# GpSimd's second-stage sums in pieces by feature block, joint scores from step 8 on, one weight rounding behind a ScalarE copy

## What is computed

```python
scores = (q @ k.T) / sqrt(64);  ret = scores * decay_mask;  x = ret @ v   # 8 batches, 8 heads, 576 positions, 64 wide
h = max(x @ w1, x @ w2, x @ w3)    # 4608 tokens, 512 -> 768
x = h @ w_out                      # 768 -> 512
a, b = x @ u1, x @ u2              # 512 -> 1024
out = (a * b) @ u3 @ u_out         # 1024 -> 512
```

## Time and profile before

| | before |
|---|---|
| median of 3 runs | 1218.41 us |
| profiled execution | 1220.39 us, span 1218.6 us |
| TensorE matmul busy | 1207.2 us, 99% |
| VectorE busy | 740.1 us, 61% |
| ScalarE busy | 487.3 us, 40% |
| GpSimd busy | 438.0 us, 36% |
| DMA | 169.66 MB, mean 139 GB/s |

### The profile page before, as it was taken

One profiled execution on the slowest core, in us unless ns is written; L12 is line 12 of the kernel. 1 busy time (PEld: TensorE's weight loads), 2 busy tenths in 40 slices (PEclk: granted clock), 3 DMA queues, 4 the chain that ended last, 5 costly groups with the idle time before them and its releaser, 6 DMA issues.

```text
span 1218.6 us, 22445 instructions
## 1 busy us (share of the span) xinstructions
PE 1207.2 (99%) x8978; PEld 1182.5 (97%) x8978; DVE 740.1 (61%) x1059; ACT 487.3 (40%) x781; POOL 438.0 (36%) x234
## 2 busy tenths in 40 slices
PE   9999999999999999999999999999999999999999
PEld 8778899999999999999999999999999999999998
DVE  5556748745454454668887776454545456876652
ACT  3434544424232322326555444242424234554451
POOL 3646745220202010063787850202020217366550
PEclk9999999999999999999999999999999999999999
DMA  9999943021212030234564531313131252444441
GB/s 360 330 354 391 310 144 136 29 85 46 78 46 85 33 98 27 83 126 147 174 227 166 169 139 53 111 52 113 57 108 64 95 190 87 155 160 158 163 155 65
DMA packets 87335, 169.66 MB, mean 139 GB/s; under 512 B 9272, under 2 KB 58680, under 8 KB 87232
## 3 DMA queue, kind: packets, MB, share of 16 engines
q1 hardware_dynamic: 87232, 168.24, 39.2%
HBM read 106.33 MB, written 61.87 MB: 138 GB/s over the span
## 4 chain that ended last, share of the span: by engine, by line
PE 95%; issue 2%; DMA 1%; DVE 1%; ACT 0%; SPq 0%; POOL 0%; DVEq 0%; ACTq 0%; POOLq 0%
PE ps L1354 28%; PE ps L1356 28%; PE ps L1355 28%; PE ps L1262 2%; PE ps L1276 1%; PE ps L1206 1%; PE ps L1249 1%; PE ps L1222 1%; PE ps L1280 1%; PE ps L1278 1%; DMA xd<-xst 1%; DMA vs<-vv 0%; PE ps L1177 0%; DMA raw<-hd 0%; DVE probs L1005 0%
## 5 line engine op out<-in xcount | busy, mean ns | idle before, releaser
L1354 PE MATMUL ps<-chi,whi 128*128 128x384 f32 x2016 | 673.9, 334 | 1.2 <-ACT w L985 0.7
L1356 PE MATMUL ps<-chi,wlo 128*128 128x384 f32 x2016 | 673.4, 334 | 0.0
L1355 PE MATMUL ps<-clo,whi 128*128 128x384 f32 x2016 | 673.4, 334 | 0.0
L724 POOL TENSOR_TENSOR raw<-raw,raw 128x768 f32<-128x768 f32 (+3 forms) x102 | 269.2, 2659 | 572.0 <-DMA raw<-xd 203.9
L1354 PEld LDWEIGHTS ps<-chi,whi 128*128 128x128 f32 x2016 | 378.4, 188 | 2.6 <-ACT w L985 1.0
L1355 PEld LDWEIGHTS ps<-clo,whi 128*128 128x128 f32 x2016 | 378.4, 188 | 0.0
L1356 PEld LDWEIGHTS ps<-chi,wlo 128*128 128x128 f32 x2016 | 378.4, 188 | 0.0
L994 DVE TENSOR_TENSOR clo<-raw,chi 128x768 fp32r<-128x768 f32 (+2 forms) x168 | 253.0, 1534 | 33.7 <-ACT chi L903 33.7
L903 ACT CAST chi<-raw 128x768 fp32r<-128x768 f32 (+2 forms) x168 | 180.3, 1082 | 83.9 <-PE ps L1356 51.0
L985 ACT COPY w<-ps 128x384 f32<-128x384 f32 x126 | 60.7, 482 | 240.9 <-PE ps L1356 239.3
L972 ACT COPY u<-ps 128x384 f32<-128x384 f32 x126 | 60.8, 483 | 161.2 <-PE ps L1356 159.6
(11 more groups left out here) (64 smaller groups left out, 796.6 us busy)
## 6 DMA issues: line engine op xcount, KB each, us to landing
gd<-h SPq DMA_DIRECT2D x96, 192.0 KB, 1.9
raw<-gd SPq DMA_DIRECT2D x24, 768.0 KB, 6.0
qks<-qk SPq DMA_DIRECT2D x30, 576.0 KB, 7.0
hd<-h SPq DMA_DIRECT2D x72, 192.0 KB, 1.9
raw<-hd SPq DMA_DIRECT2D x24, 576.0 KB, 5.6
x2d<-h SPq DMA_DIRECT2D x48, 192.0 KB, 2.7
raw<-x2d SPq DMA_DIRECT2D x24, 384.0 KB, 4.1
outT<-h SPq DMA_DIRECT2D x48, 192.0 KB, 1.9
```

The lines of the kernel that those rows point to most:

```text
L724: return nc.gpsimd.tensor_tensor(out_, a, b, op)
L1354: nc.tensor.matmul(to, w1, x1, start=(start and k == 0), stop=False, skip_group_check=True)
L1355: nc.tensor.matmul(to, w1, x2, start=False, stop=False, skip_group_check=True)
L1356: last = nc.tensor.matmul(to, w2, x1, start=False, stop=(k == KH[st] - 1), skip_group_check=True)
```

## The change

Three edits. The last four lines of each `combine` case become a helper, `pieces`, which for every tile of stage C splits each of the four sums into `KH[C]` = 3 instructions of 128x384; for the first tile of stage O the sums i = 2 and 3 stay in four pieces as they were. The semaphore counts up at the last piece. `SINGLE` goes from 4 to 8, so steps 4 to 7 use single scores, and `late_features` keeps a late feature only from step 7 on. The cast of weight 11's second part moves from "p2" to "w", behind the copy `w`.

```diff
+W_HI[11, 1] = (56, "w")
-SINGLE = 4
+SINGLE = 8
-    return features(m)[-1:] if m < STEPS - 2 else []
+    return features(m)[-1:] if SINGLE - 1 <= m < STEPS - 2 else []
+                def pieces(to, a, b):
+                    parts = KH[tau // TILES] if tau // TILES == C or (tau == O * TILES and i >= 2) else 1
+                    for k in range(parts - 1):
+                        add(x(to, k), x(a, k), x(b, k), ALU.subtract)
+                    k = slice(None) if parts == 1 else parts - 1
+                    add(x(to, k), x(a, k), x(b, k), ALU.subtract).then_inc(combined, 1)
-                    add(x(4), x(3), x(0), ALU.subtract).then_inc(combined, 1)
+                    pieces(4, 3, 0)
-                    add(x(1), x(6), x(4), ALU.subtract).then_inc(combined, 1)
+                    pieces(1, 6, 4)
...
+                    pieces(3, 6, 3)
...
+                    pieces(5, 2, 1)
```

## The result

The changed kernel takes 1234.34 us (median of 4 runs, 1233.11 to 1238.11), the kernel before 1218.61 us (4 runs, 1218.19 to 1220.7). The ratio of the runs on record is 1.0122, 95% interval 1.0105 to 1.014: slower, by 14.9 us if the ratio is taken (0.0122 x 1218.6), by 15.7 us if the medians are. The forecast was 1224.8 us, its range ended at 1228.5. The direction was right, the size was not: +15.7 us where +6.4 stood.

The account below looks back on a forecast made before the run. TensorE, 95% of the chain of waits, was taken to bound the kernel. Terms of -0.7 + 7.4 - 0.9 + 0.6 = +6.4 us on 1218.4 gave 1224.8 us; range with the rivals 1216.8 to 1228.5.

Parts of the forecast that it names:

- the chain: Tile 7: third sum ends 2.1 us later, its cast and copy `s` follow on ScalarE, TensorE stalls 1.5 us with restart.
- The turns: GpSimd and VectorE in stage C: the waiting one is served when an instruction ends; one turn costs GpSimd 1.1 us.
- The loop through `h`: Stage C: the next tile's load waits behind copy `h`; rounds become 23.7 us, +5.7 us from tile 8 to 11.
- waits of weights 12 and 13 at `w`: Expected sign in stage C: new TensorE idle times waiting for ScalarE's copy `w` at units 60 and 64.
- tiles 7 to 11, +7.4: Stage C after its first tile: pieces make sums, `s` and `u` late; +1.2 to +10.2 us, taken as +7.4.
- tile 6: First tile of stage C: pieces hold VectorE's op less and remove a 0.5 us idle time and slow restart; -0.7 us.
- Nothing on TensorE's path by my count: First tile of stage C: GpSimd's 11.51 us become some 14, which only weight 10 waits for.
- the cast of weight 11: Unit 56: `w` no longer stands behind this cast, so a 0.7 us idle time and its restart go; -0.9 us.
- the retention: Front of the kernel, `SINGLE` 8 and late features: dearer single scores against fewer stops and less half clock; +0.6 us.
- Step 6's stop: Retention: TensorE's 1.07 us stop, read as a late instruction block, goes because blocks last some 1.3 us longer; -1.07 us.
- Step 4's: Retention: TensorE's 2.44 us stop keeps its place in the stream and hides that step's +1.08 us of single scores; 0.
- The lower end of the turns: Rival for stage C: VectorE's turns fall as before, only the pieces' fixed part is paid; 1218.6 us, chance 0.24.

Follow-up runs that it names:

- scores only: Only `SINGLE` 8 and the late features changed against the kernel before, cast and sums as before: 1221.26 us, ratio 1.0006.
- tile 6 and one more sum: Changed kernel with stage C's pieces only in tile 6 and tile 7's first sum, scores and cast as changed: 1219.87 us, ratio 0.999 to the kernel before.
- cast only: Only the cast of weight 11's second part moved behind the copy `w`, against the kernel before: 1220.01 us, ratio 1.0.
- the reordered kernel: Changed kernel, all pieces kept, position 3's cast behind copy `s` and position 5's behind `h` and `u` in stage C: 1225.42 us, ratio 1.0042.
- only `h` and `u` moved: Changed kernel, all pieces kept, only position 5's cast put behind copies `h` and `u` in stage C: 1225.93 us, ratio 1.0042.

## Why the prediction was wrong in size

**Right: the chain.** The turns, who is queued behind whom, and which copy is late were as worked out. The third sum was foretold to end at 580.6 us and `s` to be there at 582.15. Tile 7 began 0.58 us later than before (568.61 for 568.03). With that added, the third sum was to end at 581.2 and `s` at 582.73; they ended at 581.16 and 582.73. The wait with its slow matmul, 1.5 foretold, was 1.4. The loop through `h` and the waits of weights 12 and 13 at `w` came as named. No idle time was left near 537 us, as foretold.

**Wrong: the term "tiles 7 to 11, +7.4".** It measured 3.8 + 1.6 + 3.1 + 2.2 + 3.3 = 14.0 us. Of the 6.6 us that it missed:
- 2.8 us was my discount. Without it the forecast would have been 1227.6 us, still 6.7 us short. The working gave 10.2, and I took 7.4 since part of the turns "may be put off". No row supported that. The turns were not put off: in tile 7 three rests were ready and went in, one for each piece.
- 1.5 us in tile 7. I counted two turns and "some 0.5" in the fourth sum. There were three: 6.40 us in place of 5.1 (2.91 + 2 x 1.1), and `u` cost 2.1 us, not 0.7 (the step in front of P7 was 1.95 us too long, the one behind it 0.1).
- 1.6 us is the half clock behind that wait. I had the row for it in the retention and never asked it of stage C, where I was adding new stops.
- 0.7 us in tiles 9 to 11: 8.6 against 7.9. A round was 24.4 us, not 23.7. The part from the first sum to the end of `h` was no longer than foretold: 16.8, 17.1 and 17.9 us in tiles 8, 9 and 10, against 17.8, with two turns in the fourth sum of tiles 9 to 11. Longer was the way from there to the next first sum, 7.5, 7.4 and 6.5 us in place of 5.9. The 5.9 was one row; the two rounds behind it in the kernel before took 7.7 and 6.5 us there. Why the load is slower at one time than at another stays open.

**Wrong: tile 6.** -0.7 foretold, +0.6 measured (1.4 against 0.8). The 0.8 us at 537 us went whole: VectorE's op there takes 0.92 us in place of 2.65. (My "held 2.1 us less" had no row behind it; beside a piece has 1.30 us.) But the four sums last 13.2 us (531.1 to 544.4) for 11.5, and further on there is new lost time: 0.3 us at 551.5 us, 0.1 at 561.2, 0.6 at 563, where one of VectorE's rests of the tile ("DVE clo") is late, and 0.3 at 570. The wait for that rest stands in six of the nine kernels with pieces in tile 6 and in none with whole sums there; the other three wait 0.3 to 0.7 us for VectorE's `w` between 550 and 555 us instead. "Nothing on TensorE's path by my count" counted only weight 10.

**Right: the cast of weight 11**, -0.9 in the trace of the changed kernel. By itself it made nothing that the runs can tell, and in its own profile the race in tile 8 took more than it gave.

**Half right: the retention.** +0.6 foretold (-1.6 to +2.7), 0 measured, +0.7 in the runs of the scores alone. Step 6's stop went, as foretold. Step 4's was to stay in its place in the stream; it did (behind 593 matmuls, as before), and was shorter, 0.62 us:

```profile
40.87 0.49 PE L1177 MATMUL ps<-qks 64*128 64x128 f32 x3 [0.62 <-issue]
```

The clock did not fall behind it. In the whole retention "issue" fell from 4.3 to 1.3 us and the 1.7 us of half clock went; against that stand 4 x 1.08 = 4.3 us of single scores and 0.8 us more of waiting for `xst`, together -3.0 - 1.7 + 4.3 + 0.8 = +0.4 us, where 0 was measured. That 0 is partly luck: among profiles of one and the same retention stage B starts at 162.2 to 167.9 us.

**What should have warned me.** The lower end of the turns was a kernel in which VectorE's ops fall as before, and I weighed it at 0.24. But VectorE in stage C is busy for 90.23 of 109 us and GpSimd for 87.76: two engines that take turns can't both have 80% of the time, their waits for each other included, and leave the other alone.

## What to carry to other kernels

Cutting an operation into pieces so that another engine gets in helps only the one that gets in; the one that was cut pays a turn for every piece as long as the other has work ready. So ask first what is queued in order behind its result. Here a cast on ScalarE waited for the cut sum, and behind it stood a copy that closes the loop to the next tile's load: the order on that queue was worth 9.8 of 14.9 us. And where a hand-worked sum comes to 10.2, take 10.2 unless a row says less.

## What the runs showed of the hardware

- **Who comes first by hundredths of a microsecond gets its turn whole.** 0.05 us behind GpSimd's sum, a VectorE rest of 128x1536 took 4.22 us (scores only); 0.10 us ahead of it (tile 6 and one more sum) and 0.23 us ahead (kernel before), 1.75 us. 0.04 us behind, a rest of 128x768 took 3.46 us (cast only), against 0.94 us where no sum ran (kernel before).
- **Stops of TensorE that nothing in the profile releases come and go between profiles.** In the three profiles with single scores up to step 3 only, TensorE stood near 40 us for 2.4, 1.9 and 2.2 us with no releaser, and again for 0.8 to 1.1 us near 67 us. In the eleven with single scores up to step 7, whose retention is the same program, the second stop never came. The first was 2.0 to 2.5 us in three, 0.6 and 0.8 in two, and absent in six. Stage B began at 166.6 to 167.9 us in the three, and at 162.2 to 164.6 us in the eight others. Further stops of 0.4 to 1.5 us lie between 85 and 146 us in eight of the eleven. So one profile can't price this stretch: the starts of stage B lie 5.7 us apart, nearly as far as the runs of one kernel.
- **Whether such a stop comes varies, where it comes does not.** The first stands behind 593 matmuls in seven of the eight profiles that have it, the later ones behind 1096, 1472 and 2225 with single scores up to step 3, and behind 1344, 1721, 2097 and 2474 with them up to step 7. From 593 on, all these distances are whole multiples of some 251 matmuls and weight loads. That is what instruction blocks of one size would give, as I had read the two stops; no run here moved a block's edge by itself. The Trainium skill ("Runtime: NRT & Kernel Launch", section "Instruction fetch mechanics") calls the crossing of an instruction block mostly hidden. If the stop near 40 us is such a crossing, six of these eleven traces agree and the three with 2.0 to 2.5 us do not.
- **The clock does not fall behind every stop.** Behind waits of 1.78 us (tile 7, changed kernel), 2.19 us (scores only) and 2.8 us (the reordered kernel) the granted clock was 0.50 for some 3.4 us; behind the four of 1.7 to 1.8 us in the kernel with the third sum whole and the two of 1.7 us with only `h` and `u` moved it stayed at 1.00.
